# A chunked linear-attention front with two feed-forward stages: decay steps written to the other of two buffers, and products grouped into fewer slots

## What is computed

```python
for t in range(S):
    kt, vt, rt, wt = (k[:, :, t], v[:, :, t], r[:, :, t], w[:, :, t])
    cur = np.einsum('bhd,bhe->bhde', u[None] * kt, vt)
    y[:, :, t] = np.einsum('bhd,bhde->bhe', rt, state + cur)
    state = wt[:, :, :, None] * state + np.einsum('bhd,bhe->bhde', kt, vt)
```

## Time and profile before

| | before |
|---|---|
| median of 3 runs | 1018.37 us (1017.75 to 1018.85) |
| the profiled execution | 1017.5 us, span 1015.7 us |
| PE busy | 994.5 us, 98% |
| DVE busy | 559.8 us, 55% |
| ACT busy | 288.6 us, 28% |
| POOL busy | 24.4 us, 2% |
| chain that ended last | PE 96%, DVE 1%, issue 1% |
| start (before the first large matmul) | 0 to 42.3 us |
| gated stage with attention phases | 42.3 to about 515 us |

### The profile page before, as it was taken

One profiled execution on the slowest core, in us unless ns is written; L12 is line 12 of the kernel. 1 busy time (PEld: TensorE's weight loads), 2 busy tenths in 40 slices (PEclk: granted clock), 3 DMA queues, 4 the chain that ended last, 5 costly groups with the idle time before them and its releaser, 6 DMA issues.

```text
span 1015.7 us, 27744 instructions
## 1 busy us (share of the span) xinstructions
PE 994.5 (98%) x11776; PEld 971.7 (96%) x11776; DVE 559.8 (55%) x1170; ACT 288.6 (28%) x604; POOL 24.4 (2%) x24
## 2 busy tenths in 40 slices
PE   5899999999999999999999999999999999999998
PEld 5799999999999999999999999999999999999998
DVE  7686655655656646556432437555545454555554
ACT  3435314223242241331222334222121222222212
POOL 4500000000000000000000000000000000000000
PEclk9999999999999999999999999999999999999999
DMA  6644401312113013110020413010101010101000
GB/s 162 167 135 120 117 14 35 109 30 64 53 29 92 25 31 91 52 38 2 26 60 1 138 35 125 1 47 1 47 1 47 1 46 0 46 4 43 15 11 24
DMA packets 42130, 52.96 MB, mean 52 GB/s; under 512 B 5152, under 2 KB 42016, under 8 KB 42016
## 3 DMA queue, kind: packets, MB, share of 16 engines
q1 hardware_dynamic: 40624, 51.04, 17.3%
q10 hardware_dynamic: 1392, 0.25, 0.2%
HBM read 39.48 MB, written 9.44 MB: 48 GB/s over the span
## 4 chain that ended last, share of the span: by engine, by line
PE 96%; DVE 1%; issue 1%; ACT 0%; ACTq 0%; DMA 0%; SPq 0%; DVEq 0%
PE products L166 18%; PE products L167 16%; PE products L168 16%; PE acc L168 12%; PE acc L166 12%; PE acc L167 12%; PE products L694 5%; PE products L736 1%; PE products L752 1%; PE products L671 1%; PE products L708 1%; PE products L721 1%; DMA x_parts<-f_y 0%; DVE k_in L927 0%; DVE a_sb L944 0%
## 5 line engine op out<-in xcount | busy, mean ns | idle before, releaser
L166 PE MATMUL products<-x_parts,weights_hi 128*128 128x384 f32 x576 | 200.9, 349 | 4.1 <-DMA x_parts<-f_y 1.9
L167 PE MATMUL products<-x_parts,weights_hi 128*128 128x384 f32 x576 | 194.2, 337 | 0.0
L168 PE MATMUL products<-x_parts,weights_lo 128*128 128x384 f32 x576 | 193.9, 337 | 0.0
L1235 DVE TENSOR_SCALAR leaky_low<-products,leaky_al 128x384 f32<-128x384 f32 x128 | 79.0, 617 | 169.4 <-PE products L168 169.3
L1095 DVE TENSOR_TENSOR g_sb<-a_g,products 128x384 f32<-128x384 f32 x96 | 53.2, 554 | 191.4 <-issue 129.5
L1182 ACT ACTIVATE leaky_g_hi<-leaky_g_sb 128x384 fp32r<-128x384 f32 x128 | 67.2, 525 | 295.0 <-DVE leaky_g_sb L1240 295.0
L514 ACT ACTIVATE g_hi<-g_sb 128x384 fp32r<-128x384 f32 x96 | 50.3, 524 | 254.1 <-DVE g_sb L1095 254.1
L166 PEld LDWEIGHTS products<-x_parts,weights_hi 128*128 128x128 f32 x576 | 108.1, 188 | 8.9 <-issue 5.3
L167 PEld LDWEIGHTS products<-x_parts,weights_hi 128*128 128x128 f32 x576 | 108.2, 188 | 0.0
L168 PEld LDWEIGHTS products<-x_parts,weights_lo 128*128 128x128 f32 x576 | 108.2, 188 | 0.0
L168 PE MATMUL acc<-g_hi,weights_lo 128*128 128x384 f32 x288 | 97.5, 338 | 0.0
(11 more groups left out here) (85 smaller groups left out, 1747.7 us busy)
## 6 DMA issues: line engine op xcount, KB each, us to landing
k_in<-in_k_dram SPq DMA_DIRECT2D x16, 336.0 KB, 3.9
r_in<-in_r_dram SPq DMA_DIRECT2D x16, 336.0 KB, 4.8
stage<-in_w_out_dram SPq DMA_DIRECT2D x14, 384.0 KB, 3.1
w_v<-in_v_dram SPq DMA_DIRECT2D x16, 288.0 KB, 3.5
y_dram<-x_in SPq DMA_DIRECT2D x8, 576.0 KB, 3.0
x_in<-y_dram SPq DMA_DIRECT2D x8, 576.0 KB, 4.4
out_dram<-leaky_out_sb SPq DMA_DIRECT2D x7, 576.0 KB, 3.3
stage<-in_w_dram SPq DMA_DIRECT2D x10, 336.0 KB, 3.8
```

Source lines behind the costliest of these rows:

```text
L166: pe.matmul(out, w_hi, x_hi, start=first, stop=False)
L167: pe.matmul(out, w_hi, x_lo, start=False, stop=False)
L168: return pe.matmul(out, w_lo, x_hi, start=False, stop=last)
L1235: dve.tensor_scalar(self.low[f % 2][:, :], h, 0.0, self.al[:, f:f + 1], ALU.min, ALU.mult).then_inc(self.low_ready, 1)
```

## The change

Keys have a second buffer, `k_scratch`, and queries `r_leaf`, for levels 2 and 4; levels 1, 3 and 5 read `k_in` and `r_in`. A step reads one buffer and writes the other, so it waits for the products of the level before the one it reads for. A step changes half of the positions; of the other half, the quarter that the next level reads and that isn't in the other buffer yet is copied by ACT (`carry_over`, two copies of 192 elements per partition for each stream, for four levels of each duo). New semaphores `k_copied` and `r_copied` tell of them.

On PE, from duo 1 on, phases 3, 5 and 9 have no slot. Levels 2 and 3 share the slot of phase 4, levels 4 and 5 that of phase 6, key values of both streams that of phase 8, and the weighted values of both streams stand in phase 10. A slot whose round before has none (phases 2, 4, 6 and 10) is placed right behind `up_a`, and waits for `g_sb` of the round before; then come `up_b` and `down`. Bank 4 is shared for every round with a slot; in a round without one the result of `up_b` goes to bank 0 or 1, and waits for what was there: for leaf merges (phases 1 and 3), for merges of level 2 (phase 5), for the states of stream 0 (phase 9).

On DVE a new `attend_before` runs ahead of `g_sb`: in phase 2 the four steps of level 1 and both merges of level 1, in phase 4 merges of level 2, in phase 5 the four steps of level 4, in phase 6 merges of level 4, in phase 10 two output parts. Behind `g_lo` are the two key steps of level 2 (phase 2), the two query steps of level 2 (phase 3), four steps of level 3 (phase 4), merges of level 3 (phase 5), and the merges of level 5, now masked and all on DVE (phase 6). `carry_states` stays where it was: stream 0 behind `g_lo` of phase 8, stream 1 behind that of phase 9. ACT copies the outputs of stream 0 ahead of `g_hi`. The start has a new order of steps and merges on DVE too.

The core of the diff:

```diff
-    return g >= 0 and step_at(g) is not None and step_at(g) % PHASES != 1
-
-
-def shared_bank(g):
-
-    return slot_at(g - 1) and slot_at(g)
+    return g >= 0 and step_at(g) is not None and step_at(g) % PHASES not in (1, 3, 5, 9)
...
+            def keys_for(j, phase):
+
+                return k_scratch[j] if phase in (2, 4) else k_in[j]
+
+            def queries_for(n, j, phase):
+
+                return r_leaf[j] if phase in (2, 4) else queries_of(n, j)
+
+            def quarter(tile, h, low, high):
+
+                return view(tile, low * h + 2 * h * high, [[4 * h, S // (4 * h)], [1, h]])
...
-                at = BANK * (4 if shared_bank(g) else g % 2)
+                at = BANK * (4 if slot_at(g) else g % 2)
...
-                def copy_last_level(n):
-
-                    for j in range(2):
-                        act.wait_ge(products_done[j], after(n, 5))
-                    act.wait_ge(merged, merges(n, 4, 0))
-                    for row0 in (0, 64):
-                        done = copy(view(a_sb, 32, [[BLOCK, 2 * CH], [1, 32]], 32, row0),
-                                    view(products, level_bank(5, 0), [[32, 2 * CH], [1, 32]], 32, row0))
-                    done.then_inc(copied, 1)
+                def carry_over(n, j, phase):
+
+                    source, to = phase, phase + 1
+                    h = 2 if phase <= 2 else 8
+                    low, high = (1, 0) if phase % 2 else (0, 1)
+                    act.wait_ge(products_done[j], after(n, phase - 1))
+                    if phase == 1:
+                        act.wait_ge(k_first[j], n + 1)
+                    else:
+                        act.wait_ge(k_stepped[j], 4 * n + phase - 1)
+                        act.wait_ge(k_copied[j], 4 * n + phase - 1)
+                    copy(quarter(keys_for(j, to), h, low, high), quarter(keys_for(j, source), h, low, high)).then_inc(k_copied[j], 1)
+                    act.wait_ge(r_stepped[j], 6 * n + phase)
+                    if phase > 1:
+                        act.wait_ge(r_copied[j], 4 * n + phase - 1)
+                    copy(quarter(queries_for(n, j, to), h, high, low),
+                         quarter(queries_for(n, j, source), h, high, low)).then_inc(r_copied[j], 1)
...
-                        copy_last_level(n)
+                    if n == 0 and phase in (0, 3, 4):
+                        carry_over(0, 0, 1 if phase == 0 else phase)
+                        if phase > 0:
+                            carry_over(0, 1, phase)
+                    elif n == 0 and phase == 1:
+                        carry_over(0, 1, 1)
+                        carry_over(0, 0, 2)
+                    elif n == 0 and phase == 2:
+                        carry_over(0, 1, 2)
+                    elif phase == 2:
+                        carry_over(n, 0, 2)
+                        carry_over(n, 1, 2)
+                    elif phase == 4:
+                        for part in (3, 4):
+                            carry_over(n, 0, part)
+                            carry_over(n, 1, part)
...
+                    if phase == 1 and n > 0:
+                        carry_over(n, 0, 1)
+                        carry_over(n, 1, 1)
...
+                    if step_at(g) is not None and step_at(g) % PHASES == 10:
+                        copy_outputs(step_at(g) // PHASES, 0)
...
-                    if phase >= 3:
-                        pe.wait_ge(merged, merges(n, phase - 2, 1))
-                    elif phase == 2 or n > 1:
-                        pe.wait_ge(merged, merges(n, 0, 5 - 2 * phase))
+                    if n == 0 and phase == 2:
+                        pe.wait_ge(merged, merges(n, 0, 1))
+                    elif n > 0 and phase == 1:
+                        pe.wait_ge(merged, merges(n, 0, 3))
+                    elif phase > 1:
+                        pe.wait_ge(merged, merges(n, phase - 2 if n == 0 else 2 * (phase // 2) - 1, 1))
                     for j in streams:
                         pe.wait_ge(r_stepped[j], 6 * n + phase)
                         if phase == 1:
                             pe.wait_ge(k_first[j], n + 1)
                         else:
                             pe.wait_ge(k_stepped[j], 4 * n + phase - 1)
+                            pe.wait_ge(k_copied[j], 4 * n + phase - 1)
+                            pe.wait_ge(r_copied[j], 4 * n + phase - 1)
...
                     else:
+                        weighted_values(n, 0)
                         weighted_values(n, 1)
...
-                    elif 2 <= phase <= 6 and step != 2:
+                    elif n == 0 and 3 <= phase <= 6:
+                        level(n, phase - 1)
+                    elif phase == 2 and n > 0:
+                        level(n, 1)
+                    elif phase in (4, 6) and n > 0:
+                        level(n, phase - 2)
                         level(n, phase - 1)
...
                         key_values(n, 0)
-                    elif phase == 9:
+                        if n > 0:
+                            key_values(n, 1)
+                    elif phase == 9 and n == 0:
                         key_values(n, 1)
                         weighted_values(n, 0)
...
-                    if shared_bank(g - 1):
+                    if slot_at(g - 1):
...
+                            n, phase = divmod(step_at(g), PHASES)
+                            if phase in (1, 3):
+                                pe.wait_ge(merged, merges(n, 0, g % 2))
+                            elif phase == 5:
+                                pe.wait_ge(merged, merges(n, 2, g % 2))
+                            elif phase == 9:
+                                pe.wait_ge(states_done[0], states_after(n))
...
+                    lone = slot_at(g) and not slot_at(g - 1)
+                    if lone:
+                        pe.wait_ge(g_ready, g)
+                        attend(step_at(g))
                     if slot_at(g - 1):
                         down(g - 1)
                     if g > 0:
                         up_b(g)
                     if g > 0 and not slot_at(g - 1):
                         down(g - 1)
-                    if slot_at(g):
+                    if slot_at(g) and not lone:
...
+                        dve.wait_ge(k_copied[j], 4 * n + level - 1)
+                    dve.wait_ge(products_done[j], after(n, level - 1))
+                    dve.tensor_tensor(halves(keys_for(j, level + 1), h, 0), halves(keys_for(j, level), h, 0), decay(n, j, h, 1),
+                                      ALU.mult).then_inc(k_stepped[j], 1)
...
+                def attend_before(step):
+                    n, phase = divmod(step, PHASES)
+                    if phase == 2:
+                        steps(n, 1)
+                        merge_levels(n, 1)
+                    elif phase == 4:
+                        merge_levels(n, 2)
+                    elif phase == 5:
+                        steps(n, 4)
+                    elif phase == 6:
+                        merge_levels(n, 4)
+                    elif phase == 10:
+                        lower_outputs(n, (0, 1))
+
+                def merge_levels(n, phase):
+
+                    merge_level(n, 0, phase)
+                    merge_level(n, 1, phase)
+
                 def attend_early(step):
                     n, phase = divmod(step, PHASES)
-                    if 2 <= phase <= 5:
-                        step_k(n, 0, phase - 1)
-                    elif phase == 6 and n > 0:
+                    if phase == 6:
                         last_step_k(n, 0)
+
+                def steps(n, level):
+
+                    for j in range(2):
+                        step_k(n, j, level)
+                    for j in range(2):
+                        step_r(n, j, level)
...
-                    elif 2 <= phase <= 5:
-                        merge_level(n, 0, phase - 1)
-                        step_k(n, 1, phase - 1)
-                        merge_level(n, 1, phase - 1)
-                        if n > 0:
-                            step_r(n, 0, phase - 1)
-                            step_r(n, 1, phase - 1)
+                    elif phase == 2:
+                        for j in range(2):
+                            step_k(n, j, 2)
+                    elif phase == 3:
+                        for j in range(2):
+                            step_r(n, j, 2)
+                    elif phase == 4:
+                        steps(n, 3)
+                    elif phase == 5:
+                        merge_levels(n, 3)
                     elif phase == 6:
-                        if n > 0:
-                            last_step_k(n, 1)
-                        copy_last_level(n)
+                        last_step_k(n, 1)
+                        merge_levels(n, 5)
...
-                merge_level(0, 0, 1)
-                merge_level(0, 1, 1)
                 step_k(0, 1, 2)
                 products_of_w(0, 0, 2, range(3, 7))
-                merge_level(0, 0, 2)
```

(33 more changed lines are left out.)

78 lines of the change are left out of this document (40 added, 38 removed).

## The result

The changed kernel takes 1083.58 us in the median (1080.85 to 1085.75), the kernel before 1018.31 us: a ratio of 1.064, 95% interval 1.0615 to 1.0665, slower by 65 us. The forecast was 1052.7 us with a range of 1041 to 1062. The profiled execution is one of 1085.75 us, with a span of 1084.0 us and a granted clock of 0.976 in the mean.

The account below looks back on a forecast made before the run. PE, at 96% of the chain, was taken as the bound. Duos 2 to 7 add 28.6 us, duo 1 6.01, the start -0.3: +34.3, giving 1052.7 us, range 1041 to 1062.

Parts of the forecast that it names:

- the clock: Rival: the clock falls behind seven gaps of 2.3 us or more, 1.7 us lost each, +12 us, 1064; chance 0.11.
- the start: Before the steady duos: 0.3 us of gain, bounds 1.5 either way; first large matmul stays at 42.
- The three waits: PE idles each duo for `g_sb`, level-3 merges and states: 2.36, 1.41 and 1.90 us.
- the walk: New DVE and PE lists placed on traced times through one duo, phase by phase, to find where PE waits.
- `g_sb`: Phase 2: four steps and two merges on DVE delay it; `up_a` of round 3 waits 2.36 us, duo 1 3.99.
- level 4: Phase 6: the shared slot behind `up_a` waits for both level-3 merges; PE idles 1.41 us a duo.
- states: Phase 10: weighted values of stream 1 wait for its states; PE idles 1.90 us a duo.
- The gain of 0.90 a duo: Three of ten slots go in duos 1 to 7, each saving 0.30 us of switching on PE.
- ACT's copies at zero: Sixteen new copies a duo on ACT cost nothing; upper bound 1.3 us a duo, 9 in all.
- The pairs don't hold together: Rival: level 3 or 5 waits inside its slot for steps or copies, up to 1 us a duo, +7, 1059; chance 0.06.
- the 96 products of a level cost 1.53 us: Price of a level's small products on PE, read from the earlier trace and used in the walk.
- Dense large matmuls surround these gaps: Argument against the clock rival: large matmuls around the new gaps speak against the clock falling there.

Follow-up runs that it names:

- e4_three: The changed kernel with level-1 steps and merges behind `g_lo` of round 2, level 4 waiting only for level-2 merges, both states carried in phase 8: 1042.40 us.
- e6_twice: The kernel before, with the products of level 2 made twice in their slot in duos 1 to 7: 1030.49 us, ratio 1.0117.
- e7_split: e4_three with levels 3 and 5 moved behind `up_b` of the same round, so each pair is parted: 1029.82 us, ratio 1.0114.
- e1_phase2: The changed kernel with four steps and two level-1 merges moved from ahead of `g_sb` of round 2 to behind that round's `g_lo`: 1061.24 us.
- e2: The changed kernel with level 4 waiting only for the merges of level 2, not those of level 3: 1069.29 us, ratio 1.0479.
- e5: The changed kernel with both level-1 merges of duo 0 ahead of the four products of decays on DVE at the start: 1084.56 us, one execution.
- e8_gap: The kernel before, with ten chained memsets of `g_sb` ahead of it in phase 2 of duos 1 to 7: 1057.23 us, ratio 1.0379.

## Why the prediction was wrong

The forecast in the sum was 34.3 us, and the profiles differ by 68.3. Three terms that the sum had at zero or near it make up most of the difference: the clock (nothing, 24 measured), idle time inside the paired slots (nothing, 9.4), and the start (-0.3, +3.1). The three waits came out 7.3 us smaller than forecast.

*Direction, and the walk: right.* All three waits stand where the walk put them, seven each. Sizes (forecast, measured): `g_sb` 2.36 and 2.09, in duo 1 3.99 and 2.5; level 4 1.41 and 1.24; states 1.90, and 1.70 in the duos with an even number, which the walk used, and 1.28 in the others. In sum 41.3 was forecast and 34.0 came. Of the 7.3 us between them, 2.5 are the odd duos (four times 0.62), for which I had used an even duo's states, and 1.5 is duo 1; the rest is a little too much on each wait. The gain of 0.90 a duo is confirmed by e4_three's clean duos (0.7 to 0.9). The Trainium skill (TensorEngine Tiling, Key Properties) says that changing the tiling mode drains TensorE; it gives no price, and the 0.30 us a slot from rows held.

*ACT's copies at zero: right.* They take 0.37 us in the mean and no wait of PE names them.

*"The pairs don't hold together": the right place, the wrong cause and price.* The rival let steps or copies be late by 1 us a duo. The steps were in time. What was late were the instructions. The step that failed was "the 96 products of a level cost 1.53 us", carried over to 192 in a row with no question whether the engine gets its instructions at that rate. The kernel before needed no such question: behind its start only one of its slots ran dry, by 0.64 us, and there the packet was late (e6_twice). Idle time inside the slots came to 9.4 us here, and e7_split, which leaves no level slot with two packet ends, removes it. That it is the supply of instructions rests on two things in the traces: a packet starts 2.3 to 2.9 us before PE goes on, each time, and where PE stops inside a level slot it is at a packet end, in every run here. No run changed the supply itself.

*The clock: at nothing in the sum, and the rival's price and place too small.* I gave it 0.11 and +12 us, behind the gaps of phase 2. It took 24. Two of those seven gaps had a stretch behind them, 3.4 us lost, and e1_phase2, without them, lost about 4 us less. The rest went mostly with the level slots: 41.0 of the 51.2 us at half clock began in or behind a level slot with idle time in it or just ahead of it, and parting the pairs left no such stretch after duo 1 (e7_split). The sign I looked for was too simple as well. "Dense large matmuls surround these gaps" was not true of the idle time at level slots, and where it was true, behind gaps of 2.1 to 2.5 us, the clock fell in 12 of 28 cases. Nor is it small products as such: none of the 28 waits of 1.28 to 1.71 us for the states in four runs (this kernel, e1, e2 and e5) had a fall behind it, though small products surround them. What decides between these cases stays open. The Trainium skill (TensorE: Matmul & The Clock Gate, Part 1) has the clock follow how busy TensorE has lately been; the runs agree in kind, in that all seven gaps of 3.3 us or more had half clock behind them (e8_gap) and shorter ones only in part.

*The start: +3.1 instead of -0.3, outside its bounds of 1.5.* I reasoned by what PE waits for between levels and did not walk VectorE's list, which puts four products of decays ahead of the merges of level 1. With two buffers GpSimd no longer waits for PE either: its steps run on from 10.9 to 17.4 us without a pause, and VectorE's own steps beside them take 1.25 us instead of the 0.47 of the earlier trace rows (0.86 at this place in the kernel before), though its merges beside them keep their 0.5. The merges of level 1 start at 20.13 instead of 17.10. The Trainium skill (SBUF — State Buffer, SBUF: two separate sides) has an exclusive port pair that a GpSimd operation and a VectorE one with two SBUF inputs take in turns; that fits, since the merges read PSUM.

## What to carry to other kernels

Putting small work together on the bounding engine saves switches that can be read off the trace (0.30 us each here), but walk the other engines' lists at the new place first: each wait that a segment of large matmuls used to cover comes back in full. Before a run of small instructions is made longer, count instructions per microsecond against what the packets of the instruction queue bring (here 256, and 3.2 to 3.7 us from one packet end to the next where PE ran dry), and look in the profile for idle time marked "issue" in the middle of a group. Price a gap with what the clock does behind it, and look at several gaps of one size and several executions: the same gaps of 2.1 us had half clock behind two, three or five of seven.

## What the runs showed of the hardware

- TensorE, at 15 ns a product with its weight load, ran dry of instructions in 7 of the 14 level slots of the changed kernel: idle 1.07 to 1.93 us, ended 2.3 to 2.9 us after a 16 KB packet of the instruction queue started. It stops at packet ends, 256 instructions apart. A level slot that contained two ends ran dry at the second, in all versions with pairs, except in duo 4, where the first end stands within a few products of the slot's start: its slot of phase 4 never ran dry, that of phase 6 not in e2_phase6 and e4_three, which don't wait ahead of it. The same edit costs nothing in one duo and 1.4 us and a clock stretch in the next.
- In seven of the ten level slots of the changed kernel that had idle spells of 1.1 to 1.9 us in or just ahead of them, 3.4 or 6.8 us at 1.2 GHz began in the slot or right behind it. Gaps of 2.1 to 2.5 us between large matmuls had such a stretch in 12 of 28 cases, gaps of 3.3 us or more in seven of seven, waits of 1.28 to 1.71 us in the middle of the slots of phase 10 in none of 28. Among those slots' gaps for instructions, 1.47 us had one (e4_three), 1.39 and 1.28 us had none (e7_split). No length of a gap alone tells them apart.
- None of the changed versions beats the kernel before; the nearest is e7_split at 1.0114.
